# A fused convolution and two feed-forward layers: the first tile's tap sums move from VectorE to TensorE

## The chip, the cores and the metric

The kernel runs on one core of one Trainium2 chip. The metric is the device time of one execution in microseconds (us), lower is better. A profiled execution also gives a span: the time from its first to its last instruction.

## What is computed

Two batches of 4096 rows with 192 channels go through a causal convolution whose seven weights are drawn for each row and each of eight heads (24 channels a head) and pass a softmax first. The result goes through two feed-forward layers of width 2048, the first with a squared ReLU, the second with `h * cos(h)`.

```python
w = exp(weight_gen - max(weight_gen, -1)); w = w / (sum(w, -1) + 1e-09)
out = np.einsum('bshk,bskhg->bshg', w, x_unf)   # x_unf: rows s-6 .. s of x, by head
x = out.reshape(8192, 192)
h = np.maximum(x @ w_in, 0.0);  x = h * h @ w_out      # first layer
h = x @ w_in2;  out = (h * np.cos(h)) @ w_out2          # second layer
```

## The kernel before

**Tiles and slots.** The 8192 tokens are worked off in 16 tiles of 512 (`TILES`, `TOK`). A tile has 16 slots (`SLOTS`), one for each 128 columns of the hidden width, so slot `n` runs from 0 to 255. The program is written out without loops on the chip: each engine has its own list of instructions, and semaphores order the engines among themselves. What stands in these lists, and where, is set by hand, by tables such as `CONV_SLOTS` and `HI_AT`.

**Precision.** Each matrix is held as a high part in float32r (TensorE's reduced float32) and a low part that is the difference. A product is then three float32r matmuls (high by high, low by high, high by low). ScalarE makes the high parts, VectorE or GpSimd the low ones. The 192 channels are split into 128 (part 0, names with `a`) and 64 (part 1, names with `d`). Most matmuls are issued as two halves, for the upper and the lower 64 rows of the array (`TOP`, `BOTTOM`, `tile 64*128` in the profile).

**The first tile's convolution** is the place of the change. On VectorE, `convolve_first` multiplies seven shifted windows of `xc` (4 rows by 192 channels = 768 elements a partition) by the weights in `gen` and adds the products up in `x1`. The seven products go by turns into four buffers: the two halves of `tap`, `relu` and `wave` (its tile is shown as `turns`). The last tap is split by channels so that part 0 is done first. TensorE has nothing to compute in this time: it runs transpositions of the identity, `keep_busy` (L621), in counts that follow VectorE's steps, then turns the finished sum with `turn_x1` (L702: 8 transpositions of 64 rows for each part) into two PSUM tiles, part 0 into `y1` and part 1 into `y2`. The semaphore `x1_turned` tells ScalarE, which makes `xa_hi` and `xd_hi` (L1245); VectorE makes `xa_lo` and `xd_lo` (L1531).

**Around it.** In the head ScalarE makes the high parts of the first four weight pieces (`piece_his`, L1100) ahead of `xa_hi`; the other twelve follow at the end of slots given by `HI_AT`. VectorE makes the low parts of piece 0 (L1523, L1527) after `convolve_first`; when both are there (`piece_ready[0]`, 2), GpSimd starts on the low parts of all other pieces (L554 to L560). SyncE loads the pieces into a ring of four stage buffers, and the rows of the second tile (`load_rows(1)`, L450) once `first_product` says that the last product has been made.

**The slots of the head.** Slots 0 to 2 are one block each (`up_alone`, six matmuls); slots 3 to 17 (`head_slot`) interleave the product into the hidden layer with the product out of it for the slot three before, for which they wait for `g1_ready`: VectorE's low part `g_lo` (L1486). In `ACT_SQUARES` ScalarE does the squaring, in the other slots VectorE. VectorE also computes the second tile's convolution (`convolve_second`, L1360 and L1369: 7 products and 6 sums) behind the work of the slots in `CONV_SLOTS`, and softmax steps behind the slots in `SOFTMAX_AFTER`. After slot 13 TensorE turns the second tile. From slot 19 on both layers run together.

Of the kernel before, what the change touches and what calls it, by code (L numbers as in the profile page):

```python
# [7 lines left out]
def conv_ffn_ffn_kernel(nc, x_d, gen_d, w_in1_d, w_out1_d, w_in2_d, w_out2_d, out_dram):  # L8
# [103 lines left out]
    with ctx:  # L112
# [82 lines left out]
        first_sum = sem("first_sum")  # L195
# [52 lines left out]
        LATE = 4  # L248

        ACT_SQUARES = (2, 3, 4, 5, 6, 7, 8)  # L250
        CONV_SLOTS = (1, 1, 2, 2, 3, 4, 5, 6, 7, 8, 9, 10, 11)
# [3 lines left out]
        HI_AT = {4: 2, 5: 4, 6: 5, 7: 6, 8: 8, 9: 9, 10: 11, 11: 13, 12: 15, 13: 18, 14: 20, 15: 22}  # L255
# [94 lines left out]
        def turn_banks(t, part):  # L350

            return y2 if (t, part) == (0, 1) else y1

# [242 lines left out]
        def _(pe):  # L596
# [91 lines left out]
            def down_d(down, side, k, start=False, stop=False):  # L688

                y, l, f, hi, lo = down  # L690
                return half(y[:, 1, :], wo[l][:, f, DA:2 * P], lo if k == 1 else hi, side, start=start and f == 0,
                            stop=stop and f == SLOTS - 1)

# [335 lines left out]
            def head_slot(t, i, par, o, down):  # L1029
# [31 lines left out]
                if (t, i) == (0, turn_at(0)):  # L1061
                    pe.wait_ge(x1_ready, 1)
# [18 lines left out]
            turn_x1(0, 1)  # L1081
# [8 lines left out]
        def _(act):  # L1090
# [180 lines left out]
        def _(dve):  # L1271
# [100 lines left out]
            def convolve_first():  # L1372

                weights = gen[:, 0:JJ * GEN].rearrange("p (r k) -> p r k", k=TAPS)
                flat = [tap[:, 0, :], tap[:, 1, :],
                        relu[:, :, :].rearrange("p b n -> p (b n)")[:, 0:JJ * DM],
                        wave.rearrange("p b n -> p (b n)")[:, 0:JJ * DM]]
                total = x1[:, 0:JJ * DM]
# [4 lines left out]

                def product(k):
                    if k >= 4:
                        dve.wait_ge(first_sum, k - 4 + (k == 4))
                    tap_k = last - k
                    dve.tensor_tensor(flat[k % 4].rearrange("p (r g) -> p r g", g=GROUP),
                                      xc[:, tap_k * DM:(tap_k + JJ) * DM].rearrange("p (r g) -> p r g", g=GROUP),
                                      weights[:, :, tap_k:tap_k + 1].to_broadcast([P, JJ * HEADS, GROUP]),  # L1390
                                      ALU.mult).then_inc(first_product, 1)

                def last_product(a, b):
                    by_head = [v.rearrange("p (j h g) -> p j h g", j=JJ, g=GROUP)[:, :, a:b, :]
                               for v in (flat[last % 4], xc[:, 0:JJ * DM])]
                    of_heads = gen[:, 0:JJ * GEN].rearrange("p (j h k) -> p j h k", j=JJ, k=TAPS)[:, :, a:b, 0:1]
                    dve.wait_ge(first_sum, last - 4)
                    dve.tensor_tensor(by_head[0], by_head[1], of_heads.to_broadcast([P, JJ, b - a, GROUP]),
                                      ALU.mult).then_inc(first_product, 1)

                def channel_sum(k, a, b):
# [171 lines left out]
```

## Time and profile before

| | |
|---|---|
| median of 3 runs | 1182.05 us (1182.01 to 1182.32) |
| the profiled execution | 1182.28 us |
| its span | 1180.5 us |
| TensorE busy, share of the span | 1163.7 us, 99% |
| VectorE | 965.2 us, 82% |
| ScalarE | 807.2 us, 68% |
| GpSimd | 366.9 us, 31% |

The profiled execution took 1.8 us more than its span, which lie before its first and behind its last instruction. It stands 0.23 us above the median of the runs. Engines are named PE (TensorE's matmuls), PEld (its weight loads, which overlap them), DVE (VectorE), ACT (ScalarE), POOL (GpSimd) and SP (SyncE); L1388 is line 1388 of the kernel. The end of a matmul is modelled, so that TensorE counts as busy in short waits too; the starts of its instructions say more than its busy time.

### The profile page before, as it was taken

How to read it: one execution, taken by the hardware profiler on the slowest of the kernel's cores; microseconds unless marked ns; L12 is line 12 of the kernel's file. 1: busy time of each engine (PE TensorE's matmuls, PEld its weight loads, DVE VectorE, ACT ScalarE, POOL GpSimd, SP SyncE). 2: the span in 40 equal slices, each digit the busy share in tenths (PEclk: the TensorE clock that was granted, in tenths of full speed). 3: DMA queues.
4: the chain of work that ended last, by engine and by line, in shares of the span. 5: the costliest groups of instructions: out<-in, count | busy, mean ns of one | idle time of the engine just before them, and what ended most of it. 6: DMA issues, size and time to landing. Idle time of an engine off the chain costs nothing.

```text
span 1180.5 us, 25485 instructions
## 1 busy us (share of the span) xinstructions
PE 1163.7 (99%) x9800; PEld 1120.5 (95%) x9800; DVE 965.2 (82%) x1506; ACT 807.2 (68%) x1467; POOL 366.9 (31%) x265
## 2 busy tenths in 40 slices
PE   6999999999999999999999999999999999999998
PEld 5889999999999999999999999999999999999976
DVE  7978899978878787787878878787787878878787
ACT  4887666767666676676766666676676667666675
POOL 3995524070430706125070430705115070000000
PEclk9999999999999999999999999999999999999999
DMA  7512111011111101111011111101111000100000
GB/s 188 140 50 48 35 28 35 15 27 27 24 35 28 35 9 20 34 28 34 15 19 34 24 35 28 35 9 21 34 28 34 14 16 4 25 2 14 1 15 15
DMA packets 113173, 37.32 MB, mean 32 GB/s; under 512 B 101662, under 2 KB 110878, under 8 KB 113052
## 3 DMA queue, kind: packets, MB, share of 16 engines
q1 hardware_dynamic: 111100, 34.87, 14.1%
q8 instruction: 79, 1.29, 0.5%
q10 hardware_dynamic: 1952, 0.80, 0.3%
q14 instruction: 42, 0.34, 0.1%
HBM read 23.84 MB, written 6.29 MB: 26 GB/s over the span
## 4 chain that ended last, share of the span: by engine, by line
PE 92%; POOL 3%; DVE 2%; ACT 1%; issue 1%; SPq 0%; DMA 0%; POOLq 0%; ACTq 0%; DVEq 0%
PE y L600 48%; PE h L600 43%; POOL wd_lo L556 1%; POOL wa_lo L554 1%; POOL wo L560 1%; POOL wo L558 0%; DVE x L1414 0%; DMA xc<-in_x_dram 0%; POOL gen L540 0%; DVE turns L1323 0%; ACT relu L1116 0%; DVE x L1403 0%; DVE xd_lo L1510 0%; DVE g_lo L1328 0%; DVE h L1335 0%
## 5 line engine op out<-in xcount | busy, mean ns | idle before, releaser
L600 PE MATMUL y<-g_hi,wo 64*128 64x512 f32 x3048 | 693.0, 393 | 0.2
L600 PE MATMUL y<-g_lo,wo 64*128 64x512 f32 x2032 | 514.3, 392 | 0.0
L600 PEld LDWEIGHTS y<-g_hi,wo 64*128 64x128 f32 x3048 | 412.5, 184 | 16.3 <-PE y L600 4.9
L521 POOL TENSOR_TENSOR tap<-xc,gen 128x768 f32<-128x768 f32 x98 | 151.0, 1547 | 575.1 <-DVE xd_lo L1492 559.3
L600 PEld LDWEIGHTS y<-g_lo,wo 64*128 64x128 f32 x2032 | 295.6, 184 | 1.9
L1141 ACT ACTIVATE turns<-turns 128x512 f32<-128x512 f32 x238 | 150.5, 633 | 182.6 <-DVE turns L1443 182.6
L600 PE MATMUL h<-xa_hi,wa_hi 64*128 64x512 f32 x1018 | 264.7, 395 | 0.6 <-DVE g_lo L1486 0.4
L600 PE MATMUL h<-xa_lo,wa_hi 64*128 64x512 f32 x1018 | 262.8, 393 | 0.4 <-DVE g_lo L1328 0.3
L600 PE MATMUL h<-xa_hi,wa_lo 64*128 64x512 f32 x1018 | 261.5, 391 | 0.0
L1463 DVE TENSOR_TENSOR h<-h,turns 128x512 f32<-128x512 f32 x238 | 165.7, 696 | 114.9 <-ACT turns L1141 114.5
L1437 DVE SCALAR_TENSOR_TENSOR h<-h,relu 128x512 f32<-128x512 f32 x249 | 173.4, 696 | 56.6 <-ACT relu L1116 54.2
L1154 ACT ACTIVATE g_hi<-h 128x512 fp32r<-128x512 f32 x238 | 142.9, 600 | 86.8 <-DVE h L1463 86.8
L1116 ACT ACTIVATE relu<-h 128x512 f32<-128x512 f32 x256 | 152.8, 597 | 65.6 <-PE h L600 65.0
L1473 DVE SCALAR_TENSOR_TENSOR g_lo<-h,g_hi 128x512 fp32r<-128x512 f32 x238 | 164.7, 692 | 19.1 <-ACT g_hi L1154 0.9
L1486 DVE TENSOR_TENSOR g_lo<-h,g_hi 128x512 fp32r<-128x512 f32 x256 | 174.4, 681 | 1.6 <-issue 0.7
L1443 DVE SCALAR_TENSOR_TENSOR turns<-h,turns 128x512 f32<-128x512 f32 x238 | 162.3, 682 | 0.9 <-ACT turns L1126 0.5
L1166 ACT ACTIVATE g_hi<-relu 128x512 fp32r<-128x512 f32 x256 | 158.3, 618 | 0.4
L600 PEld LDWEIGHTS h<-xa_lo,wa_hi 64*128 64x128 f32 x1018 | 147.9, 184 | 3.7 <-DVE g_lo L1328 1.6
L600 PEld LDWEIGHTS h<-xa_hi,wa_lo 64*128 64x128 f32 x1018 | 148.1, 184 | 0.7
L1126 ACT ACTIVATE turns<-h 128x512 int32<-128x512 f32 x238 | 141.8, 596 | 1.4 <-PE h L600 1.4
L600 PEld LDWEIGHTS h<-xa_hi,wa_hi 64*128 64x128 f32 x1018 | 128.6, 184 | 12.5 <-issue 2.2
L600 PE MATMUL h<-xd_hi,wd_hi 64*128 64x512 f32 x513 | 132.6, 392 | 0.0
(122 smaller groups left out, 1067.1 us busy)
## 6 DMA issues: line engine op xcount, KB each, us to landing
xc<-in_x_dram SPq DMA_DIRECT2D x60, 240.0 KB
out_dram<-arena SPq DMA_DIRECT2D x62, 64.0 KB, 1.9
xt_a<-x_blocks SPq DMA_DIRECT2D x224, 16.0 KB, 1.8
arena<-in_moe_w_out_dram SPq DMA_DIRECT2D x16, 192.0 KB, 3.3
arena<-in_moe_w_in_dram SPq DMA_DIRECT2D x16, 128.0 KB, 2.6
out_dram<-arena SPq DMA_DIRECT2D x62, 32.0 KB, 1.7
xt_d<-x_blocks SPq DMA_DIRECT2D x112, 16.0 KB, 1.8
arena<-in_moe_w_in_dram SPq DMA_DIRECT2D x16, 64.0 KB, 2.9
```

The source lines that it names most:

```text
L521: pool.tensor_tensor(tap[:, k % 2, :].rearrange("p (r g) -> p r g", g=GROUP), rows[k], wk, ALU.mult).then_inc(pool_step, 1)
L600: return pe.matmul(o, w[rows, :], x[rows, :], start=start, stop=stop)
L1116: act.activation(relu[:, b, :], h1_bank(n), ACT.Relu).then_inc(relu_done, 1)
L1126: act.activation(turns[:, c, :], h2[c], ACT.Copy, bias=0.25).then_inc(turns_ready, 1)
L1141: act.activation(wave[:, c, :], wave[:, c, :], ACT.Sin, scale=2.0 * math.pi).then_inc(cos_ready, 1)
L1154: act.activation(g2_hi[:, c, :], h2[c], ACT.Copy, scale=2.0 * math.pi).then_inc(g2_hi_ready, 1)
L1166: act.activation(g1_buffers(n)[0], relu[:, n % 2, :], ACT.Square).then_inc(g1_hi_ready, 1)
L1437: dve.scalar_tensor_tensor(h1_bank(n), h1_bank(n), 0.0, relu[:, b, :], ALU.max, ALU.mult).then_inc(square_ready, 1)
L1443: dve.scalar_tensor_tensor(wave[:, c, :], h2[c], 0.25, turns[:, c, :], ALU.add, ALU.subtract).then_inc(fraction_ready, 1)
L1463: dve.tensor_tensor(h2[c], h2[c], wave[:, c, :], ALU.mult).then_inc(g2_made, 1)
L1473: dve.scalar_tensor_tensor(g2_lo[:, c, :], h2[c], 2.0 * math.pi, g2_hi[:, c, :], ALU.mult, ALU.subtract).then_inc(g2_ready, 1)
L1486: dve.tensor_tensor(lo, h1_bank(n), hi, ALU.subtract).then_inc(g1_ready, 1)
```

## The change

1. VectorE no longer adds in the first tile: `convolve_first` makes only the products (eight instructions in place of fifteen; the last tap is still split into the first 144 and the last 48 channels). It waits for `first_taken`, which TensorE raises when a tap's buffer has been read.
2. TensorE sums: `sum_x1` multiplies each product block by the identity with true float32 operands and accumulates the seven taps in PSUM, 16 matmuls for a tap, in place of `turn_x1` for this tile and of 55 of the `keep_busy` transpositions. 18 `keep_busy` transpositions are issued as soon as the first softmax maximum is there.
3. ScalarE makes the last of piece 2's and all of piece 3's high parts behind `xa_hi` and `xd_hi`.
4. `CONV_SLOTS` starts the second tile's convolution in slot 3 in place of slot 1 and ends it in slot 10 in place of 11, with two steps a slot up to slot 7. `HI_AT` moves pieces 4 to 7 from slots 2, 4, 5, 6 to slots 4, 5, 6, 7.

```diff
-        CONV_SLOTS = (1, 1, 2, 2, 3, 4, 5, 6, 7, 8, 9, 10, 11)
-        HI_AT = {4: 2, 5: 4, 6: 5, 7: 6, 8: 8, 9: 9, 10: 11, 11: 13, 12: 15, 13: 18, 14: 20, 15: 22}
+        WARM_UP = 18
+        CONV_SLOTS = (3, 3, 4, 4, 5, 5, 6, 6, 7, 7, 8, 9, 10)
+        HI_AT = {4: 4, 5: 5, 6: 6, 7: 7, 8: 8, 9: 9, 10: 11, 11: 13, 12: 15, 13: 18, 14: 20, 15: 22}
...
+            def sum_x1(k, part):
+
+                for jj in range(JJ):
+                    at = jj * DM + part * DA
+                    for side in range(2):
+                        rows = slice(side * DD, (side + 1) * DD)
+                        o = turn_banks(0, part)[0:DD if part else P, side, part * TOK // 2:(part + 1) * TOK // 2].rearrange(
+                            "p (q j n) -> p j q n", j=JJ, n=BLOCK)
+                        x = first_buffer(k)[rows, at:at + (DD if part else DA)]
+                        last = pe.matmul(o[:, jj], x, ident[rows, rows], start=k == 0 and jj == 0,
+                                         stop=k == TAPS - 1 and jj == JJ - 1)
+                return last
...
-            for k in range(2):
+            pe.wait_ge(gen_max[0], 1)
+            keep_busy(WARM_UP)
+            for k in range(TAPS):
                 pe.wait_ge(first_product, k + 1)
-                keep_busy(8 - k)
-            for k in range(1, TAPS - 2):
-                pe.wait_ge(first_sum, k)
-                keep_busy(8)
-            keep_busy(6)
-            pe.wait_ge(first_sum, TAPS - 1)
-            turn_x1(0, 0)
-            keep_busy(2)
-            pe.wait_ge(first_sum, TAPS + 1)
-            pe.wait_ge(pad_zeroed, 1)
-            turn_x1(0, 1)
+                last = sum_x1(k, 0)
+                if k == TAPS - 1:
+                    last.then_inc(x1_turned, 1)
+                    pe.wait_ge(first_product, k + 2)
+                last = sum_x1(k, 1)
+                last.then_inc(x1_turned if k == TAPS - 1 else first_taken, 1)
...
-            for pc in range(RING):
+            for pc in range(2):
                 for op in range(3):
                     piece_his(pc, op)
+            for op in range(2):
+                piece_his(2, op)
             for part in range(2):
                 act.wait_ge(x1_turned, part + 1)
                 act.activation(by_half(x1_high(0, part)), x1_source(0, part), ACT.Copy).then_inc(x1_hi_ready, 1)
+            piece_his(2, 2)
+            for op in range(3):
+                piece_his(3, op)
...
+                dve.wait_ge(x_own, FIRST_OWN)
+                product(0, 0, HEADS)
+                dve.wait_ge(x_loaded, FIRST_X)
+                for k in range(1, last):
                     if k >= 4:
+                        dve.wait_ge(first_taken, k - 3)
+                    product(k, 0, HEADS)
+
+                dve.wait_ge(first_taken, last - 3)
+                product(last, 0, wide)
+                product(last, wide, HEADS)
```

The order of the instructions shows it at three places. On VectorE, the first tile's convolution, before (`tap`, `relu` and `turns` are the product buffers, `x` is the sum `x1`):

```order
L1388 TENSOR_TENSOR relu<-xc,gen 128x768
L1414 TENSOR_TENSOR x<-tap 128x768
L1388 TENSOR_TENSOR turns<-xc,gen 128x768
L1414 TENSOR_TENSOR x<-x,relu 128x768
L1388 TENSOR_TENSOR tap<-xc,gen 128x768
L1414 TENSOR_TENSOR x<-x,turns 128x768
L1388 TENSOR_TENSOR tap<-xc,gen 128x768
L1414 TENSOR_TENSOR x<-x,tap 128x768
L1398 TENSOR_TENSOR relu<-xc,gen 128x4x144
L1403 TENSOR_TENSOR x<-x,tap 128x4x128
L1398 TENSOR_TENSOR relu<-xc,gen 128x4x48
L1403 TENSOR_TENSOR x<-x,relu 128x4x128
```

And in the changed kernel, the whole of it with the four instructions behind it:

```order
L1408 TENSOR_TENSOR tap<-xc,gen 128x768 x2
L1408 TENSOR_TENSOR relu<-xc,gen 128x768
L1408 TENSOR_TENSOR turns<-xc,gen 128x768
L1408 TENSOR_TENSOR tap<-xc,gen 128x768 x2
L1408 TENSOR_TENSOR relu<-xc,gen 128x4x144
L1408 TENSOR_TENSOR relu<-xc,gen 128x4x48
L1516 TENSOR_TENSOR wa_lo<-arena,wa_hi 128x256
L1520 TENSOR_TENSOR wd_lo<-arena,wd_hi 64x256
L1524 TENSOR_TENSOR xa_lo<-y,xa_hi 128x512
L1524 TENSOR_TENSOR xd_lo<-y,xd_hi 64x512
```

All sums are gone, and the low parts of weight piece 0 follow the last product at once. On TensorE, from the program's start to the first matmul of slot 0, before:

```order
L621 MATMUL h<-ident 128x128 x53
L702 MATMUL y<-ident,x 128x2x32 x8
L621 MATMUL h<-ident 128x128 x2
L702 MATMUL y<-ident,x 128x2x32 x8
L628 MATMUL h<-xa_hi,wa_hi 128x512
```

and in the changed kernel:

```order
L628 MATMUL h<-ident 128x128 x18
L711 MATMUL y<-ident,tap 128x2x32 x8
L711 MATMUL y<-ident,tap 64x2x32 x8
L711 MATMUL y<-ident,tap 128x2x32 x8
L711 MATMUL y<-ident,tap 64x2x32 x8
L711 MATMUL y<-ident,relu 128x2x32 x8
L711 MATMUL y<-ident,relu 64x2x32 x8
L711 MATMUL y<-ident,turns 128x2x32 x8
L711 MATMUL y<-ident,turns 64x2x32 x8
L711 MATMUL y<-ident,tap 128x2x32 x8
L711 MATMUL y<-ident,tap 64x2x32 x8
```

(two more taps of 16 matmuls follow before slot 0). The last place is VectorE in slots 3 to 5 of the changed kernel, where `tap` and `y` belong to the second tile's convolution, `stat` to the softmax and `g_lo` is what TensorE waits for:

```order
L1384 TENSOR_TENSOR tap<-xc,gen 128x768 x2
L1300 TENSOR_REDUCE stat<-gen 128x64
L1479 TENSOR_TENSOR g_lo<-h,g_hi 128x512
L1393 TENSOR_TENSOR y<-tap 128x768
L1384 TENSOR_TENSOR tap<-xc,gen 128x768
L1300 TENSOR_REDUCE stat<-gen 128x64
L1479 TENSOR_TENSOR g_lo<-h,g_hi 128x512
L1393 TENSOR_TENSOR y<-y,tap 128x768
L1384 TENSOR_TENSOR tap<-xc,gen 128x768
L1300 TENSOR_REDUCE stat<-gen 128x64
```

Before, the first four of the convolution's steps stood behind slots 1 and 2, and from slot 3 on each slot had one. The lists of GpSimd and SyncE are the same in both kernels.

## Rows read from the trace of the kernel before

**Rows 1.** The page: busy time of two engines, and the chain that ended last.

```profile
PE 1163.7 (99%) x9800; PEld 1120.5 (95%) x9800; DVE 965.2 (82%) x1506; ACT 807.2 (68%) x1467; POOL 366.9 (31%) x265
PE 92%; POOL 3%; DVE 2%; ACT 1%; issue 1%; SPq 0%; DMA 0%; POOLq 0%; ACTq 0%; DVEq 0%
```

**Rows 2.** Timeline of VectorE, 0 to 24 us: start, time, instruction, idle before.

```profile
6.73 0.96 DVE L1388 TENSOR_TENSOR tap<-xc,gen 128x768 f32<-128x768 f32 x1
8.25 0.96 DVE L1388 TENSOR_TENSOR tap<-xc,gen 128x768 f32<-128x768 f32 x1 [0.57 <-DMA xc<-in_x_dram]
9.13 0.95 DVE L1388 TENSOR_TENSOR relu<-xc,gen 128x768 f32<-128x768 f32 x1
10.00 0.95 DVE L1414 TENSOR_TENSOR x<-tap 128x768 f32<-128x768 f32 x1
...
16.08 0.75 DVE L1398 TENSOR_TENSOR relu<-xc,gen 128x576 f32<-128x576 f32 x1
16.75 0.69 DVE L1403 TENSOR_TENSOR x<-x,tap 128x512 f32<-128x512 f32 x1
17.35 0.35 DVE L1398 TENSOR_TENSOR relu<-xc,gen 128x192 f32<-128x192 f32 x1
...
19.61 0.42 DVE L1527 TENSOR_TENSOR wd_lo<-arena,wd_hi 64x256 fp32r<-64x256 f32 x1
20.06 0.69 DVE L1531 TENSOR_TENSOR xa_lo<-y,xa_hi 128x512 fp32r<-128x512 f32 x1
```

**Rows 3.** Timeline of TensorE's matmuls, 7 to 24 us.

```profile
18.36 0.46 PE L702 MATMUL y<-ident,x 64*128 64x64 f32 x8 [0.40 <-DVE x L1403]
...
19.61 0.50 PE L628 MATMUL h<-xa_hi,wa_hi 128*128 128x512 f32 x1
...
20.80 0.50 PE L635 MATMUL h<-xa_lo,wa_hi 128*128 128x512 f32 x1
...
21.81 0.39 PE L600 MATMUL h<-xd_lo,wd_hi 64*128 64x512 f32 x1
```

**Rows 4.** Timeline of TensorE's weight loads, 7 to 14 us: the idle-time transpositions.

```profile
7.80 3.00 PEld L621 LDWEIGHTS h<-ident 128*128 128x128 f32 x15 [7.80 <-issue]
11.00 0.86 PEld L621 LDWEIGHTS h<-ident 128*128 128x128 f32 x8 [0.21 <-DVE x L1414]
```

**Rows 5.** Timeline of ScalarE, 0 to 24 us.

```profile
17.08 0.51 ACT L1100 ACTIVATE wo<-arena 128x384 fp32r<-128x384 f32 x1
18.87 0.60 ACT L1245 ACTIVATE xa_hi<-y 128x512 fp32r<-128x512 f32 x1 [1.27 <-PE y L702]
19.73 0.59 ACT L1245 ACTIVATE xd_hi<-y 64x512 fp32r<-64x512 f32 x1 [0.26 <-PE y L702]
22.24 0.60 ACT L1116 ACTIVATE relu<-h 128x512 f32<-128x512 f32 x1 [1.92 <-PE h L600]
```

**Rows 6.** Windows: us, busy and count of PE, PEld, DVE, ACT, POOL, clock, DMA.

```profile
44.00:48.00 4.00, 4.00 (x33) 3.67 (x30) 3.96 (x6) 3.33 (x7) 3.73 (x4) 1.00 0.56 164
```

**Rows 7.** Timeline of weight loads, 24 to 84 us: the same load in slots 9 and 10; the stall.

```profile
33.82 0.18 PEld L600 LDWEIGHTS h<-xa_hi,wa_hi 64*128 64x128 f32 x1 [0.78 <-DVE g_lo L1486]
...
41.39 0.18 PEld L600 LDWEIGHTS h<-xa_hi,wa_hi 64*128 64x128 f32 x1
...
43.96 0.18 PEld L600 LDWEIGHTS h<-xa_hi,wa_hi 64*128 64x128 f32 x1
```

**Rows 8.** Timeline of VectorE, 20 to 84 us: convolution, softmax and low part in the head.

```profile
31.62 1.37 DVE L1360 TENSOR_TENSOR tap<-xc,gen 128x768 f32<-128x768 f32 x1
...
35.51 0.94 DVE L1360 TENSOR_TENSOR tap<-xc,gen 128x768 f32<-128x768 f32 x1
36.37 0.61 DVE L1276 TENSOR_REDUCE stat<-gen 128x64 f32<-128x448 f32 x1
36.90 0.68 DVE L1486 TENSOR_TENSOR g_lo<-h,g_hi 128x512 fp32r<-128x512 f32 x1
```

**Rows 9.** Timeline of GpSimd, 20 to 84 us.

```profile
20.11 0.73 POOL L554 TENSOR_TENSOR wa_lo<-arena,wa_hi 128x256 fp32r<-128x256 f32 x1 [17.53 <-DVE wd_lo L1527]
...
27.66 1.27 POOL L556 TENSOR_TENSOR wd_lo<-arena,wd_hi 64x256 fp32r<-64x256 f32 x1
...
30.73 1.45 POOL L554 TENSOR_TENSOR wa_lo<-arena,wa_hi 128x256 fp32r<-128x256 f32 x1
```

More of the change, by code:

```diff
@@ L194, in conv_ffn_ffn_kernel @@
         first_product = sem("first_product")
-        first_sum = sem("first_sum")
+        first_taken = sem("first_taken")
         pool_step = sem("pool_step")
@@ L352, in turn_banks, with first_buffer @@
             return y2 if (t, part) == (0, 1) else y1
+        def first_buffer(k):
+            return [tap[:, 0, :], tap[:, 1, :], relu[:, :, :].rearrange("p b n -> p (b n)")[:, 0:JJ * DM],
+                    wave.rearrange("p b n -> p (b n)")[:, 0:JJ * DM]][k % 4]
         def x1_source(t, part):
@@ L1061, in head_slot @@
                 if (t, i) == (0, turn_at(0)):
+                    pe.wait_ge(pad_zeroed, 1)
                     pe.wait_ge(x1_ready, 1)
@@ L1372, in convolve_first @@
             def convolve_first():
[L1374 to L1378, printed above, removed]
                 last = TAPS - 1
                 wide = -(-DA // GROUP)
-                def product(k):
-                    if k >= 4:
[L1386 to L1399, printed above, removed]
@@ L1401, in channel_sum @@
-                def channel_sum(k, a, b):
-                    sums, more = [v.rearrange("p (j d) -> p j d", j=JJ)[:, :, a:b] for v in (total, flat[k % 4])]
-                    dve.tensor_tensor(sums, sums, more, ALU.add).then_inc(first_sum, 1)
-                dve.wait_ge(x_own, FIRST_OWN)
-                product(0)
-                dve.wait_ge(x_loaded, FIRST_X)
-                product(1)
-                for k in range(1, last - 1):
-                    product(k + 1)
-                    dve.wait_ge(first_product, k + 1)
-                    if k >= 2:
-                        dve.wait_ge(first_sum, k - 1)
-                    dve.tensor_tensor(total, flat[0] if k == 1 else total, flat[k % 4],
-                                      ALU.add).then_inc(first_sum, 1)
@@ L1417, in convolve_first @@
-                last_product(0, wide)
-                dve.wait_ge(first_product, last)
-                dve.wait_ge(first_sum, last - 2)
-                channel_sum(last - 1, 0, DA)
-                last_product(wide, HEADS)
-                dve.wait_ge(first_product, last + 1)
-                dve.wait_ge(first_sum, last - 1)
-                channel_sum(last, 0, DA)
-                channel_sum(last - 1, DA, DM)
-                dve.wait_ge(first_product, last + 2)
-                dve.wait_ge(first_sum, last + 1)
@@ L1428, in convolve_first, with product @@
-                channel_sum(last, DA, DM)
+                def product(k, a, b):
+                    tap_k = last - k
+                    to, rows = [v.rearrange("p (j h g) -> p j h g", j=JJ, g=GROUP)[:, :, a:b, :]
+                                for v in (first_buffer(k), xc[:, tap_k * DM:(tap_k + JJ) * DM])]
+                    weights = gen[:, 0:JJ * GEN].rearrange("p (j h k) -> p j h k", j=JJ, k=TAPS)
+                    dve.tensor_tensor(to, rows, weights[:, :, a:b, tap_k:tap_k + 1].to_broadcast([P, JJ, b - a, GROUP]),
+                                      ALU.mult).then_inc(first_product, 1)
```

## The prediction

> **What bounds the kernel now.** I read the page first: TensorE is busy for 99% of the span and carries 92% of the chain that ended last [rows 1]. So in the steady part only matmuls count, and this change removes none there. What it can move is the time at which that part begins. The timelines of the first 24 us show this stretch: VectorE runs without a gap from 8.25 us to beyond 19 us, seven products and their sums of 0.87 us each by their starts [rows 2], and the first matmul of slot 0 stands at 19.61 [rows 3]. From slot 3 on the same weight load comes every 2.57 us (41.39 and 43.96), with one stall of 0.78 us at 33.8, put down to `g_lo` of VectorE [rows 7]. In this stretch TensorE issues 33 half matmuls in 4.00 us, one each 0.121 us, and VectorE is busy for 3.96 of the 4 [rows 6]. So an earlier slot 0 is worth its full amount at the end, less what VectorE then fails to follow. A measurement of this kernel can tell about 0.2% (2.4 us) from no change.
>
> **The products, without the sums.** VectorE's first product ends at 7.69 (6.73 + 0.96); the second has to wait for rows of `x` and starts at 8.25 [rows 2]. The others follow at 0.87 us, which is the distance of the starts 9.13 and 10.00. With only products left, products 2 to 6 end at 9.21, 10.08, 10.95, 11.82 and 12.69, the first part of the last (0.75 us) at about 13.35, its second part at 13.65. TensorE's wait is then on these.
>
> **The sums on TensorE.** A tap is 16 float32 matmuls of 64 columns. The trace has no float32 product; it has its neighbour, the transposition of the same block by the same identity: 8 in 0.46 us with the last one's end of 0.22 us in it [rows 3], thus one each 31 to 34 ns, upper and lower half side by side. That is the bound from below. Bound from above: nothing side by side, each product as dear as two 128-wide transpositions at 0.86 / 8 = 0.107 us [rows 4], 214 ns. I take 61 ns, twice the neighbour. The product has the neighbour's operands, halves and output; what it adds is the multiplication of full float32 values, which I price as the neighbour once again, since it is nearer to that row than to one which uses all 128 rows of the array. 61 ns is also what 256 columns of a half matmul cost in the head (0.121 us for 512 [rows 6]).
>
> The Trainium skill says in "FP8 and Floating Point Precision", section "TensorE Precision Notes", that true float32 takes four passes through the array. As an estimate from it: four passes of 64 columns are 256 columns, 61 ns at the head's rate; if each pass costs a whole transposition's 31 ns, 124 ns, and the sum below would be +2.2 us in place of -3.8. No run shown here has such a product.
>
> At 61 ns a tap takes 0.98 us, a little more than VectorE's 0.87. Tap 0 runs from 7.75 to 8.73; tap 1 waits for its product and runs from 9.27; then they stand back to back: tap 5 ends at 14.17, part 0 of tap 6 at 14.66, part 1 at 15.15. With 0.2 us for the last matmul's end, `xa_hi` starts on ScalarE at 14.9 instead of 18.87 [rows 5]: **4.0 us earlier**. VectorE's waits for `first_taken` come to nothing: product 4 needs tap 0's buffer (8.9), it would start at 10.87 anyway; products 5 and 6 need 10.4 and 11.4, for starts at 11.73 and 12.60.
>
> **Slot 0.** Before, `xa_lo` started only at 20.06, behind `wd_lo` (19.61) [rows 2], though `xa_hi` had ended at 19.47. Now both low parts of piece 0 are made from 13.65 to 14.6, ahead of it, so `xa_lo` starts at 15.55 and the third matmul at about 16.3 instead of 20.80 [rows 3]. `xd_hi` follows at 15.45 to 16.05, `xd_lo` ends at 16.85, and the last matmul of the slot starts at about 17.1 instead of 21.81: another 0.7 us. The first `relu` of 22.24 [rows 5] comes at 17.5: **4.7 us earlier**. ScalarE's four moved copies (0.31 to 0.41 us by their starts, about 1.45 us) fit between 16.05 and 17.5, and the last of them used to end at 17.59 [rows 5], so their data is there.
>
> **The clock.** The first 15 transpositions took 3.00 us, 200 ns each; the next 8 took 0.86 us, 107 ns each [rows 4]. The first were at TensorE's lower level of 1.2 GHz, the next at 2.4 GHz, though nothing but transpositions had run since 7.80; the clock column of the windows prints 1.00 everywhere and does not show it. Now 18 of them start at 3.8, when the first maximum is ready, and end at 3.8 + 18 x 0.21 = 7.6, just before tap 0. The rise came by 3.2 us after the first; here that is by 7.0. I cost the clock at nothing; the cover is these 3.8 us.
>
> **SyncE and GpSimd.** The second tile's rows were issued at the end of the last product (17.70); they now stand behind the second softmax load, from about 14.3 on, and are needed only in slot 3, at about 26. GpSimd's list starts after `wd_lo`: at 14.6 instead of 20.11 [rows 9]. Both are worth nothing: none of TensorE's waits of the head was put down to GpSimd. Piece 4's high part moves from slot 2 to slot 4, so GpSimd can start on it at about 29 and has it by 32.5; TensorE wants it in slot 8, at 34. The cover is 1.5 us.
>
> **VectorE in slots 3 to 10.** Here something is paid back. The second tile's convolution now begins two slots later and ends one earlier. In slots 3 to 7 VectorE has in each slot `g_lo` (0.60 by starts), two steps of the convolution (2 x 0.87) and one maximum (0.53), 2.87 us against TensorE's 2.57. That is 1.5 us of lag after five slots. A product can also be stretched while GpSimd runs: one took 1.37 us and a like one 0.94, and GpSimd's `wd_lo` and `wa_lo` took 1.27 and 1.45 us beside 0.73 [rows 8, 9]. With 0.4 us more on three to five products the lag is 2.7 to 3.6 us. TensorE bears 2.6 us of it: a slot's `g_lo` is made 2.5 us after the slot (relu, square, low part), and wanted two slots, 5.14 us, after it. So stalls of 0 to 2.1 us come in slots 9 to 13 (the upper end has all seven products stretched and ScalarE's copies in five slots running late). Against it stands the stall of 0.78 us at 33.8, which goes, since the `g_lo` of slot 3 no longer waits behind the convolution. I take a net loss of 0.9 us; the bounds are a gain of 0.8 and a loss of 2.1.
>
> The Trainium skill, "SBUF — State Buffer", section "Who interferes with whom", has the rule that a VectorE tensor_tensor with two SBUF inputs and a GpSimd read shut each other out, the later one waiting for the whole of the first. The rows 1.37 against 0.94 agree that there is a price but show only half a product of it, so the sum keeps 0.4 us; by the rule it would be up to 0.95 for each, and the loss would pass 2.1 us.
>
> **The sum**: 4.7 - 0.9 = 3.8 us less. The profiled execution of 1182.28 us stands 0.23 us over the median of 1182.05, so I forecast 1182.05 - 3.8 = **1178.3 us**. A product's price moves this by 0.088 us a ns (taps 1 to 5 and half of tap 6, 88 matmuls behind 9.27), from 95 ns on by 0.104 (tap 0 then outlasts 9.27, and 104 matmuls stand behind 7.75): the gain falls under 0.2% at 77 ns, is gone at 103 ns, and turns to a loss over 0.2% at 126 ns.
>
> **Rivals.**
> - *TensorE becomes the bound of the sum.* The passes of a product, or its two halves, do not run side by side: 124 ns (four times the transposition's spacing) gives part 0 done at 7.75 + 104 x 0.124 = 20.6 instead of 14.6: -3.8 + 6.0 = +2.2, 1184.2 us. For it: if a product is several passes, they all go to one half before the other half's follow, where the transpositions alternate. Against it: with 512 columns the halves do overlap all through the head [rows 6]. Prices from 77 to 126 ns, chance 0.25, all within 0.2%.
> - *Slower.* The same place, the price at its upper bound: 214 ns, 3.4 us a tap, part 0 done at 7.75 + 104 x 0.214 = 30.0, 15.4 us after my 14.6: -3.8 + 15.4 = +11.6, 1193.6 us. It decides against the change from 126 ns on. Against it: halves would have to lose all overlap, which no row shows. Chance 0.14, and 0.02 for a new wait behind the moved steps.
> - *VectorE's lag eats the gain.* Stretched products in all slots: 2.1 us or more lost, 1179.5 to 1180.5 us. Chance 0.07, within 0.2%.
> - *The low clock stays during the first taps.* If the transpositions did not count, tap 0 and most of tap 1 would run at 1.2 GHz, at double price, until about 3 us after 7.75: tap 1 ends at 11.1 in place of 10.25, 0.9 us lost, 1179.2 us, still faster. Chance 0.06. The Trainium skill, "TensorE: Matmul & The Clock Gate", Part 4, says that transpose mode does not count as busy for the clock; the halved times of rows 4 speak against it.
>
> **How the numbers follow.** My forecast has 0.46. Faster: 0.46 + 0.06 = 0.52. Within 0.2%: 0.25 + 0.07 = 0.32. Slower: 0.16. The range starts at 1176.8: VectorE is the bound at its 0.87 us (a price of 54 ns or less), 5.5 us won at the first `relu`, 0.3 lost. It ends at 1184.3, which takes in the first rival at 124 ns and leaves out the slower case.
>
> **What would show it.** Right: taps of about 1 us on TensorE from 7.75 on, `xa_hi` near 14.9, the first `relu` near 17.5, then slots of 2.57 us with at most a microsecond of waits for `g_lo` around slots 9 to 13. Wrong: VectorE waiting for TensorE between products, groups of 8 sums that take 0.8 us or more, transpositions still at 200 ns when tap 0 begins, or waits of TensorE for GpSimd's low parts in slot 8.

## The result, and the profile after

| | before | changed |
|---|---|---|
| median, us | 1182.25 (7 runs, 1181.89 to 1182.39) | 1193.15 (7 runs) |
| its runs, us | one group | 1183.70, 1183.91; 1193.02, 1193.15, 1193.49, 1193.68, 1193.91 |
| ratio | | 1.0071, interval 1.0048 to 1.0094 |
| profiled execution, us (span) | 1182.28 (1180.5) | 1183.70 (1181.9) |

The forecast was 1178.3, range 1176.8 to 1184.3: the median lies outside, on the side of the slower rival. (The ratio goes by all runs of both kernels; that of the two medians is 1.0092.) The runs of the changed kernel fall into two groups 9.7 us apart, which are followed one by one below: the lower (1183.8, +1.6 us) is the one that was profiled, the upper (1193.5, +11.2 us) has no trace of its own.

The page's busy times, and its chain by engine:

```profile
PE 1170.1 (99%) x9971; PEld 1124.2 (95%) x9971; DVE 959.8 (81%) x1498; ACT 805.5 (68%) x1467; POOL 364.9 (31%) x265
PE 94%; POOL 2%; ACT 2%; DVE 1%; issue 1%; DMA 0%; ACTq 0%; POOLq 0%
```

Against [rows 1] TensorE has 6.4 us more of work and VectorE 5.4 us less. The timeline of TensorE's matmuls, 3 to 24 us (columns as in [rows 3]):

```profile
3.88 3.83 PE L628 MATMUL h<-ident 128*128 128x128 f32 x18 [3.88 <-DVE stat L1300]
7.74 3.37 PE L711 MATMUL y<-ident,tap 64*128 64x64 f32 x64
11.04 1.72 PE L711 MATMUL y<-ident,relu 64*128 64x64 f32 x32
12.69 1.72 PE L711 MATMUL y<-ident,turns 64*128 64x64 f32 x32
14.34 3.37 PE L711 MATMUL y<-ident,tap 64*128 64x64 f32 x64
17.64 1.72 PE L711 MATMUL y<-ident,relu 64*128 64x64 f32 x32
19.54 0.47 PE L635 MATMUL h<-xa_hi,wa_hi 128*128 128x512 f32 x1 [0.18 <-ACT xa_hi L1266]
...
20.32 0.48 PE L642 MATMUL h<-xa_lo,wa_hi 128*128 128x512 f32 x1
...
21.31 0.39 PE L607 MATMUL h<-xd_lo,wd_hi 64*128 64x512 f32 x1
```

The seven taps stand back to back, 1.65 us from one start to the next (11.04, 12.69, 14.34). Each shows 32 matmuls, not 16: a float32 product is recorded as two loads and two matmuls. So a product costs 1.65 / 16 = 0.103 us. By form, the groups of weight loads in 7 to 20 us (busy us, mean ns of one):

```profile
L711 PEld LDWEIGHTS y<-ident,tap 64*128 64x128 f32 x64 | 3.9, 187 | 0.5 <-DVE tap L1408 0.3
L711 PEld LDWEIGHTS y<-ident,tap 64*64 64x64 f32 x64 | 2.2, 134 | 0.3
```

The loads of part 0 (128 columns as weights) take 187 ns, those of part 1 (64) 134 ns. VectorE, 6 to 21 us:

```profile
6.73 0.96 DVE L1408 TENSOR_TENSOR tap<-xc,gen 128x768 f32<-128x768 f32 x1
7.95 0.96 DVE L1408 TENSOR_TENSOR tap<-xc,gen 128x768 f32<-128x768 f32 x1 [0.26 <-DMA xc<-in_x_dram]
...
12.81 1.03 DVE L1408 TENSOR_TENSOR relu<-xc,gen 128x576 f32<-128x576 f32 x2 [0.43 <-PE y L711]
...
14.28 0.42 DVE L1520 TENSOR_TENSOR wd_lo<-arena,wd_hi 64x256 fp32r<-64x256 f32 x1
19.43 0.69 DVE L1524 TENSOR_TENSOR xa_lo<-y,xa_hi 128x512 fp32r<-128x512 f32 x1 [4.73 <-ACT xa_hi L1266]
```

VectorE is through at 13.8 and with the low parts at 14.7, as foreseen, and then stands for 4.73 us: TensorE has become the bound of the sum. ScalarE's `xa_hi` starts at 18.80 (18.87 before, [rows 5]), the third matmul at 20.32 (20.80), the first `relu` at 21.74 (22.24). The start is won by 0.5 us, not 4.7. Two of the forecast's signs of being wrong are here: part 0's group of 8 sums takes 0.89 us, and VectorE waits for TensorE between products (0.43 us at 12.81).

Then it is paid back. TensorE's weight loads, 24 to 100 us, that waited for another engine's data in the second tile's slots:

```profile
43.80 0.18 PEld L607 LDWEIGHTS h<-xa_hi,wa_hi 64*128 64x128 f32 x1 [1.00 <-DVE g_lo L1479]
47.04 0.18 PEld L607 LDWEIGHTS h<-xa_hi,wa_hi 64*128 64x128 f32 x1 [0.85 <-DVE g_lo L1479]
49.92 0.18 PEld L607 LDWEIGHTS h<-xa_hi,wa_hi 64*128 64x128 f32 x1 [0.49 <-DVE g_lo L1479]
52.71 0.18 PEld L607 LDWEIGHTS h<-xa_hi,wa_hi 64*128 64x128 f32 x1 [0.40 <-DVE g_lo L1479]
```

Together 2.7 us, at slots 9 to 12; the stall of 0.78 us at 33.8 [rows 7] is gone. VectorE is behind since the second tile's convolution; two of its rounds:

```profile
37.54 1.49 DVE L1384 TENSOR_TENSOR tap<-xc,gen 128x768 f32<-128x768 f32 x1
38.96 0.61 DVE L1300 TENSOR_REDUCE stat<-gen 128x64 f32<-128x448 f32 x1
39.49 0.67 DVE L1479 TENSOR_TENSOR g_lo<-h,g_hi 128x512 fp32r<-128x512 f32 x1
40.09 0.95 DVE L1393 TENSOR_TENSOR y<-y,tap 128x768 f32<-128x768 f32 x1
40.95 1.50 DVE L1384 TENSOR_TENSOR tap<-xc,gen 128x768 f32<-128x768 f32 x1
```

One such slot takes 40.95 - 37.54 = 3.41 us against TensorE's 2.57, with the product stretched from 0.94 [rows 8] to 1.49. Of the seven products, four took 1.37 to 1.50 us (34.26 to 44.36) and one 1.17. The `relu` starts give the account against before, us: slot 0 -0.50, slot 6 (35.89 against 36.72) -0.83, slot 10 (46.70, 46.99) -0.29, slot 11 +0.39, slot 13 (56.64, 55.15) +1.49, last slot +1.45. The two profiled executions differ by 1.42.

So three questions are left: whether the price of the products is the whole reason for the start, whether the lag comes from the slot tables alone, and what the upper group is.

### The profile page after: what moved, and what is told of

It is laid out like the page before. It is cut to its first block, busy times and chain, and to the rows that moved or that the text cites. A ratio compares the mean times of both kernels' runs of the same rounds, so it can differ in the third digit from the quotient of the medians.

```text
span 1181.9 us, 25812 instructions
## 1 busy us (share of the span) xinstructions
PE 1170.1 (99%) x9971; PEld 1124.2 (95%) x9971; DVE 959.8 (81%) x1498; ACT 805.5 (68%) x1467; POOL 364.9 (31%) x265
## 4 chain that ended last, share of the span: by engine, by line
PE 94%; POOL 2%; ACT 2%; DVE 1%; issue 1%; DMA 0%; ACTq 0%; POOLq 0%
PE y L607 49%; PE h L607 44%; PE y L711 1%; POOL wd_lo L563 0%; POOL wo L565 0%; POOL wo L567 0%; POOL wa_lo L561 0%; PE h L628 0%; ACT relu L1135 0%; POOL gen L547 0%; DVE turns L1347 0%; DMA gen<-in_weight_gen_dram 0%; DVE xd_lo L1503 0%; DVE g_lo L1352 0%; ACT gen L1124 0%
## 5 line engine op out<-in xcount | busy, mean ns | idle before, releaser
L607 PE MATMUL y<-g_lo,wo 64*128 64x512 f32 x2032 | 507.6, 392 | 0.0
L607 PEld LDWEIGHTS y<-g_hi,wo 64*128 64x128 f32 x3048 | 404.6, 184 | 17.0 <-PE y L607 4.9
L607 PEld LDWEIGHTS y<-g_lo,wo 64*128 64x128 f32 x2032 | 287.3, 184 | 2.5
L607 PE MATMUL h<-xa_hi,wa_hi 64*128 64x512 f32 x1018 | 260.9, 395 | 1.3 <-DVE g_lo L1479 1.0
L607 PE MATMUL h<-xa_lo,wa_hi 64*128 64x512 f32 x1018 | 258.8, 393 | 0.3 <-DVE g_lo L1352 0.3
L607 PE MATMUL h<-xa_hi,wa_lo 64*128 64x512 f32 x1018 | 257.3, 391 | 0.0
L607 PEld LDWEIGHTS h<-xa_lo,wa_hi 64*128 64x128 f32 x1018 | 144.0, 184 | 3.9 <-DVE g_lo L1352 1.7
L607 PEld LDWEIGHTS h<-xa_hi,wa_lo 64*128 64x128 f32 x1018 | 144.2, 184 | 0.9
```

The costliest lines, as they stand in the source:

```text
L607: return pe.matmul(o, w[rows, :], x[rows, :], start=start, stop=stop)
```

## The experiments

Where a kernel has two groups, lower is compared with lower, by their medians. On the chips of the experiments the kernel before had medians of 1181.85 to 1182.12.

### The change unaltered, with more runs

> The changed kernel once more, unaltered. Its runs fall in two groups, near 1183.8 and near 1193.4 us, 9.6 us apart. Theory C (clock): in the upper group TensorE's clock has not risen when the sums begin at 7.7 us, so that a tap takes 3.3 us in place of 1.65 and the seven taps end near 29 in place of 19.4. Rival S (elsewhere): the 9.6 us lie behind the head, in a late landing or a wait. C expects about 7 runs in 10 near 1193.4 and, if the profiled one is of that group, taps of 3.3 us and everything behind them shifted by one amount; S expects taps of 1.65 us in every profile.

Measured: eight runs of 1183.10 to 1183.93, two of 1193.45 and 1193.98; ratio 1.0031, interval 1.0008 to 1.0054. The two groups are there on another chip, in other shares (2 of 10 in the upper one, 5 of 7 in the result), and the median depends on the shares. The lower group's median is 1183.5 here.

The profiled run is of the lower group again, so it cannot decide between the two explanations of the upper one. But its first taps differ from those above:

```profile
3.91 4.07 PE L628 MATMUL h<-ident 128*128 128x128 f32 x18 [3.91 <-DVE stat L1300]
7.92 3.67 PE L711 MATMUL y<-ident,tap 64*128 64x64 f32 x64
```

The transpositions stand 0.213 us apart to the last one here, the pace of 1.2 GHz, and the first two taps last 3.67 us in place of 3.37: the products reach their faster pace only at about 8.6 us, inside the first tap. So the forecast's sign "transpositions still at 200 ns when tap 0 begins" is met in a run of the lower group. The first `relu` comes at 22.21: of the 0.5 us won at the start 0.03 is left. The time is the same all the same (1183.66 against 1183.70): the four waits for `g_lo` are as long as above, and the 0.5 us is made up where the third tile begins. There the change's profiled run waits 1.02 us for VectorE, and this one does not:

```profile
73.80 0.19 PEld L635 LDWEIGHTS h<-xa_hi,wa_hi 128*128 128x128 f32 x1 [1.02 <-DVE xd_lo L1503]
```

### Twice the idle transpositions

```diff
-        WARM_UP = 18
+        WARM_UP = 36
```

> 36 idle transpositions ahead of the sums in place of 18: they last from 3.9 to about 10 or 11 us, and the first sum begins there instead of at 7.7. C, if only the length of the stretch ahead matters: the clock is up before the first tap in every run, all runs in one group, the sums end 2.5 to 3.5 us later than in the profiled run of the change, 1186 to 1187.5 us. C with the addition that sums do not raise the clock and transpositions do only by chance: still two groups. S: two groups 9.6 us apart at the same share as before, both 3 us higher.

Measured: 1185.89 to 1186.84, one group. The taps run from 10.95 to 22.57 and the first `relu` comes at 24.94, 3.2 us later than in the change, and the time is 3.1 us more (1186.6 against 1183.5). None of the four runs lies near 1193, and what the start loses is lost at the end.

### The slot tables of before

```diff
-        CONV_SLOTS = (3, 3, 4, 4, 5, 5, 6, 6, 7, 7, 8, 9, 10)
+        CONV_SLOTS = (1, 1, 2, 2, 3, 4, 5, 6, 7, 8, 9, 10, 11)
-        HI_AT = {4: 4, 5: 5, 6: 6, 7: 7, 8: 8,
+        HI_AT = {4: 2, 5: 4, 6: 5, 7: 6, 8: 8,
```

> The change with the slot tables of before (CONV_SLOTS from slot 1, HI_AT with pieces 4 to 7 at slots 2, 4, 5, 6). Theory V (VectorE's lag): the three waits for g_lo near 43.8, 47.0 and 49.9 (2.3 us together) go, one of about 0.8 us may come back near slot 6, and the lower group falls from 1183.7 to 1181.8 to 1182.3. Rival L: the waits come from the whole of VectorE's work in the head and stay in another place; the lower group stays within 0.5 us of 1183.7.

Measured: nine runs of 1180.73 to 1181.69, one of 1191.06. Lower group 1181.3 against 1183.5: the tables cost 2.2 us. The three largest waits of TensorE's loads, 19 to 100 us, of this kernel (in total, times, longest):

```profile
PEld h L607 <- issue: 3.1, 10, 0.5
PEld h L635 <- issue: 1.4, 4, 0.4
PEld y L657 <- DVE g_lo L1479: 0.5, 1, 0.5
```

### The slot tables of the change, alone in the kernel before

The same two lines the other way round, in the kernel before.

> The kernel before with the change's two slot tables alone; its convolution as before, first relu unchanged near 22.2. Theory (VectorE's lag in slots 9 to 13 is from the tables, 2.0 to 2.3 us, and a start 0.5 us earlier hides none of it): 1183.8 to 1184.5, with PEld waits for g_lo of the second tile in slots 9 to 12. Rival (the tables pay where the head starts later and only the sums' new load on GpSimd and ScalarE makes the lag): 1181.6 to 1182.3, no such waits.

Measured: 1183.46 to 1184.37, median 1183.79 against 1182.12; ratio 1.0016, interval 1.0007 to 1.0025. Its largest wait in the same stretch:

```profile
PEld h L600 <- DVE g_lo L1486: 2.8, 4, 1.0
```

The same four waits, without a product on TensorE. The lag is the tables' alone, 1.7 us here and 2.2 us in the change; it is no price of an earlier start. Which of the two tables makes it was not tried.

### The products as transpositions

```diff
-                        last = pe.matmul(o[:, jj], x, ident[rows, rows], start=k == 0 and jj == 0,
-                                         stop=k == TAPS - 1 and jj == JJ - 1)
+                        last = pe.transpose(o[:, jj], x, ident[rows, rows])
```

This leaves the summing out: the first tile's `x1` is then its last tap alone.

> Each float32 product of the sums is issued as a transposition of the same block (nothing is accumulated: the result of the first tile is the last tap alone). Theory P (price): 16 of them take 0.5 to 0.6 us in place of 1.65, TensorE waits for VectorE, the first half of x is ready near 13.9 and xa_hi starts near 14.2 instead of 18.8; slot 0 ends 4.5 us or more earlier, and the time falls to about 1179 to 1180 us if the waits in slots 9 to 12 stay, with one group, since at a low clock the transpositions cost only 1 us a tap. Rival: the sums are held by something else than the price of a product (semaphore, PSUM bank); then a tap stays near 1.6 us.

Measured: 1178.15 to 1179.81, median 1178.47; ratio 0.9972, interval 0.9961 to 0.9983. TensorE's matmuls:

```profile
9.75 0.68 PE L711 MATMUL y<-ident,relu 64*128 64x64 f32 x16 [0.18 <-DVE relu L1407]
...
12.36 0.69 PE L711 MATMUL y<-ident,tap 64*128 64x64 f32 x16 [0.19 <-DVE tap L1407]
13.02 0.69 PE L711 MATMUL y<-ident,relu 64*128 64x64 f32 x16
14.60 0.47 PE L635 MATMUL h<-xa_hi,wa_hi 128*128 128x512 f32 x1 [0.89 <-ACT xa_hi L1265]
```

A tap of 16 transpositions takes 0.66 us (12.36 to 13.02), recorded as 16 matmuls, not 32, and TensorE waits for VectorE at nearly every tap; the first `relu` comes at 16.87, 4.87 us before the change's, and the time is 5.0 us less (1178.5 against 1183.5). With all else of the change in place, the price of the product is what kept the start from coming early. It also gives the row that the trace of before lacked: 0.66 / 16 = 41 ns a transposition in whole taps, where I had 31 to 34.

### No idle transpositions

```diff
-        WARM_UP = 18
+        WARM_UP = 0
```

> The change without any idle transposition ahead of the sums. Theory C (clock): sums of this kind do not raise TensorE's clock in the time they take, only what stood ahead of them did. Then every run has taps of 3.3 us, xa_hi starts near 30 and the time is 1193 to 1195 us in one group, which is the change's upper group made on purpose. Rival R: sums raise the clock like any work; then the first two taps are slow, the others 1.65 us, and the time is 1185.5 to 1187 us.

Measured: 1193.24, 1197.07, 1197.28, 1197.35. The profiled run is the one of 1193.24, at the level of the upper group:

```profile
7.83 5.96 PE L711 MATMUL y<-ident,tap 64*128 64x64 f32 x64 [7.83 <-DVE tap L1408]
13.73 3.02 PE L711 MATMUL y<-ident,relu 64*128 64x64 f32 x32
...
25.52 3.02 PE L711 MATMUL y<-ident,relu 64*128 64x64 f32 x32
28.46 0.79 PE L635 MATMUL h<-xa_hi,wa_hi 128*128 128x512 f32 x1
29.05 0.63 PE L638 MATMUL h<-xa_hi,wa_lo 128*128 128x512 f32 x1
...
31.22 0.39 PE L607 MATMUL h<-xd_hi,wd_lo 64*128 64x512 f32 x1
```

A tap takes 2.95 us, start to start, at the level of 1.2 GHz; the 512-column matmul that follows takes 0.63 us, and 0.39 from 31.22 on, which is 2.4 GHz. The sums ran without a gap from 7.83 to 28.5 and the level did not rise; it rose between 30.68 and 31.22, while the fourth matmul of 512 columns ran, behind the first three and three transpositions. (The clock column of the windows prints 1.00 all through this stretch; the change of pace shows the level.) So in this trace the sums do not bring the level, and in the change only the 18 transpositions ahead of them can; that every tap of the upper group then takes 2.95 us is inferred. Here the first `relu` comes at 31.88, 10.1 us after the change's, and the time is 9.7 us more than 1183.5: the distance of the groups. One group at 1193 to 1195 was expected; the three runs near 1197 have no trace, and what cost them 4 us more is open.

### 24 transpositions, from the start of TensorE's work

```diff
-            pe.wait_ge(gen_max[0], 1)
             keep_busy(WARM_UP)
```

with `WARM_UP = 24`.

> The change with 24 idle transpositions that start as soon as the identity is there (2.6 us) in place of 18 from 3.9 us; they end at the same time, 7.7 us, so no sum is later. C: a stretch 1.2 us longer catches the rise in more runs: at most 1 in 10 in the upper group near 1193.5, the others at 1183 to 1183.8. If the share of the upper group stays as it was (8 of 17), the length of the stretch is not what decides.

Measured: all 11 runs in 1182.98 to 1184.08; ratio 1.0012, interval 1.0004 to 1.0021. The transpositions run from 2.63 to 8.01, and the first tap starts 0.2 us later than in the change. The upper group is gone, at no cost. The upper group had 7 of the 17 runs so far (the expectation says 8). Over all kernels whose products have 128 and 64 weight columns by turns: with 18 transpositions (the change twice, with the old tables, and with five blocks, below) 11 of 39 runs lie 9 us or more above their lower group, with 24 or 36 of them none of 34. That is what a missed rise would do. The margin is small even so: read from the pace of the instructions, the rise came about 3 to 6 us after the first transposition in the 13 profiles that have them, and in this run about when the first product began. In the lower group of the change nothing was to be won by this, and nothing was.

### 64 columns by 64 throughout

Part 0's product of 128 columns is split in two; slot tables of before.

```diff
-                        x = first_buffer(k)[rows, at:at + (DD if part else DA)]
-                        last = pe.matmul(o[:, jj], x, ident[rows, rows], start=k == 0 and jj == 0,
-                                         stop=k == TAPS - 1 and jj == JJ - 1)
+                        for c in range(1 if part else 2):
+                            x = first_buffer(k)[rows, at + c * DD:at + (c + 1) * DD]
+                            oc = o[c * DD:(c + 1) * DD]
+                            last = pe.matmul(oc[:, jj], x, ident[rows, rows], start=k == 0 and jj == 0,
+                                             stop=k == TAPS - 1 and jj == JJ - 1)
```

> The change with the slot tables of before, and the 128 channels of part 0 summed as two products of 64 columns in place of one of 128: 24 products a tap in place of 16. In the changed kernel's trace a product with 128 weight columns takes 0.111 us, one with 64 takes 0.058, and 0.35 us a tap pass between the groups of 128 and of 64. Theory W (weight load in series with the pass for 128 columns, and a gap where the width changes): 24 x 0.058 = 1.4 us a tap and no gap, 0.25 us a tap less, 1179.3 to 1179.9 us in the lower group against 1181.2 of the run with the old tables. If column halves also run beside each other, 0.7 to 0.9 us a tap, VectorE is the bound and the time is 1176 to 1177.5 us. Rival: a product costs 0.1 us whatever its width, 2.5 us a tap, 1187 us or more.

Measured: seven runs of 1178.55 to 1179.76, five of 1183.77 to 1187.56. TensorE's rows where one tap gives way to the next:

```profile
11.47 0.27 PE L713 MATMUL y<-ident,turns 64*64 64x64 f32 x1
...
12.40 0.27 PE L713 MATMUL y<-ident,tap 64*64 64x64 f32 x1
```

By all runs the ratio is 0.9997: no gain. A tap is now 24 products in 0.93 us (11.47 to 12.40), 39 ns each, near to VectorE's 0.87. The 1176 to 1177.5 us that were expected for such taps did not come even in the lower group. So what was dear was not a float32 product as such, but the one with weights of 128 columns, and the change of width twice a tap. The profiled run is one of 1185.35; its windows from 16 us on (columns as in [rows 6]):

```profile
16.00:20.00 4.00, 2.72 (x30) 1.84 (x24) 1.38 (x2) 2.49 (x6) 3.86 (x7) 0.97 1.06 255
20.00:24.00 4.00, 4.00 (x9) 2.11 (x8) 2.73 (x6) 1.72 (x4) 3.57 (x7) 0.50 1.03 222
24.00:28.00 4.00, 4.00 (x15) 2.66 (x15) 3.14 (x5) 2.04 (x5) 0.61 (x1) 0.50 1.13 226
28.00:32.00 4.00, 4.00 (x17) 3.33 (x17) 3.19 (x3) 2.08 (x6) 2.74 (x3) 0.50 1.10 226
```

The level, up since the first products (8.0 us), falls between 19.6 and 19.9 us, and the first slots run at 0.50. Here it was lost, not missed (of the other four runs of the upper group there is no trace). And the sums have two holes without a visible releaser, one of 0.84 us at 13.74 and one in the last tap:

```profile
17.75 0.33 PE L713 MATMUL y<-ident,relu 64*64 64x64 f32 x3 [1.28 <-issue]
```

### VectorE adds two pairs of taps, TensorE sums five blocks

Slot tables of before.

```diff
+                def add(to, more, a, b):
+                    sums, others = [first_buffer(k).rearrange("p (j d) -> p j d", j=JJ)[:, :, a:b] for k in (to, more)]
+                    dve.tensor_tensor(sums, sums, others, ALU.add).then_inc(first_product, 1)
...
+                add(3, 4, 0, DM)
...
+                add(1, 2, 0, DA)
+                add(1, 2, DA, DM)
...
-            for k in range(TAPS):
-                pe.wait_ge(first_product, k + 1)
+            BLOCKS = ((0, 1), (1, 2), (2, 3), (3, 6), (1, 9))
+            for k, (_, made) in enumerate(BLOCKS):
+                pe.wait_ge(first_product, made)
```

> The change with the slot tables of before, and two of the six additions given back to VectorE (taps 3 and 4, and 5 and 6), so that TensorE sums five blocks in place of seven. Theory B (TensorE is the bound of the sum at 1.65 us a block): its last block is fed at 14.8 and part 0 is there at 15.8 in place of 19, 3 us earlier; 1178.3 to 1179 us in the lower group; in the upper group five blocks at 3.3 us, 6.6 us more. Rival: VectorE's waits for the buffers eat it, 1180 us or more.

Measured: nine runs of 1178.52 to 1180.44, three of 1189.47 to 1190.18. The sums end at 16.89 instead of 19.36, and the first `relu` comes at 19.27, 2.5 us before the change's; the lower group's median is 1178.85. By all runs the ratio is 0.9999. The upper group does not come out of the pace of the sums: five blocks at 2.95 in place of 1.65 us are 6.5 us more, and it lies 11.1 us above the lower one. It has no trace; what the other 4.6 us are is open.

### The two better kernels with the level held

The last two kernels with 24 early transpositions, and more between the sums: one behind each tap of the first and six behind its last, two and six in the second.

> The sums with products of 64 columns by 64 throughout, the slot tables of before, 24 transpositions from the start of TensorE's work (as in early24), one more behind each tap and six behind the last. Theory (only transpositions and 512-column matmuls hold the clock, products do not): the 2.4 GHz level stays from before the first tap to the first 512-column matmul, a tap takes about 0.93 us, first relu near 18.5 to 19.5, time 1177.5 to 1179.2 in all runs, no run near 1184. Rival (the sums lose the clock whatever stands between them): two groups as in quad, 1178.5 to 1179.8 and 1183.8 to 1187.6, and a granted clock of 0.50 in some stretch between 16 and 32 us. Second rival (the transpositions stand in the sums' way): one group near 1180.5.

> hybrid (VectorE adds two pairs of taps, TensorE sums five blocks, slot tables of before) with 24 early transpositions, two more behind each block and six behind the last. Theory: one group at hybrid's lower level, 1178.5 to 1179.5, the 1190 runs gone, first relu near 19.3. Rival (the clock is lost during the sums whatever stands between them): some runs remain near 1190.

Measured: the first 1179.39 to 1180.90 and one run of 1183.09, median 1180.42, ratio 0.9987 (0.9978 to 0.9996); the second 1179.76 to 1180.36 in all 11 runs, median 1179.96, ratio 0.9983 (0.9974 to 0.9992). No run lies at 1184 or above, but both are slower than expected (1177.5 to 1179.2 and 1178.5 to 1179.5), since the transpositions lie on the path: in the second the first `relu` comes at 20.70, 1.43 us later than without them. In the first the hole is there again, on the path in the last tap:

```profile
18.04 0.68 PE L713 MATMUL y<-ident,relu 64*64 64x64 f32 x15 [1.28 <-issue]
```

### Early transpositions alone

The kernel of five blocks with the 24 early transpositions and none between.

> hybrid with the 24 early transpositions alone, none between the blocks and none behind the last. Theory (the level of 2.4 GHz is missed at the start or not at all; once it is there the sums of five blocks, 9 us long, do not lose it): one group at hybrid's lower level, 1178.3 to 1179.3, 1.0 to 1.5 us below hybrid_warm, whose 16 added transpositions lie on the path. Rival (in hybrid the level is lost during the sums, and the transpositions between the blocks were what held it): runs near 1184 to 1190 come back.

Measured: seven runs of 1178.47 to 1179.17 and one of 1184.52, median 1178.71; ratio 0.9971, interval 0.9960 to 0.9983: by its median the fastest kernel that does the whole sum, 3.4 us below before, with one run in eight above before. The one run of 1184.52 is the profiled one, and shows the level lost during the sums:

```profile
12.95 1.72 PE L711 MATMUL y<-ident,turns 64*128 64x64 f32 x32 [0.19 <-DVE turns L1413]
15.41 2.73 PE L711 MATMUL y<-ident,tap 64*128 64x64 f32 x32 [0.74 <-DVE tap L1413]
```

```profile
12.00:16.00 4.00, 3.07 (x60) 2.66 (x60) 3.97 (x6) 1.62 (x5) 0.00 (x0) 0.97 0.77 226
16.00:20.00 4.00, 4.00 (x34) 3.31 (x32) 1.82 (x4) 2.41 (x6) 3.23 (x6) 0.50 1.07 233
```

A block of the same size takes 1.72 us at the upper level and 2.73 us as the level falls. The theory's time was met in seven runs, the rival's in one.

## Why the prediction was wrong

- **The product's price** failed, and with it the forecast. "I take 61 ns, twice the neighbour": it measured 103 ns on average. In its lower group, which lies inside the range, the kernel is the first rival, TensorE as the bound of the sum, though not by halves that don't overlap: part 0's eight products stand at 111 ns each, part 1's eight at 58, and the rest of the 1.65 us (1.65 - 0.89 - 0.46 = 0.30) is at the two changes of width. My 61 was right for part 1; I took both parts as equal, though part 0's weights have 128 columns, and left out the switches. The four passes that the Trainium skill gives a true float32 product ("FP8 and Floating Point Precision", section "TensorE Precision Notes") made an estimate of 61 ns too, by their columns; part 1's 58 agrees with it, part 0's 111 does not come out of it.
- **The working from a price to the start** holds: at 103 ns it puts `xa_hi` at about 18.7, and it came at 18.80, 0.07 us earlier than before. The forecast called 103 ns neutral for the whole time, and that failed: at this price the lower group is 1.6 us slower, for the smaller win in slot 0 and the larger lag below.
- **Slot 0** was right in kind: the low parts made ahead win 0.43 us beyond `xa_hi` (0.50 - 0.07; 0.7 was said). So was the schedule of VectorE (13.8 against 13.65). The products as transpositions put the first `relu` at 16.87 where 17.5 was forecast.
- **VectorE's lag** was right in place and cause, and too small: net 1.95 us (from -0.50 to +1.45) against 0.9, within its bounds of -0.8 to 2.1. "0.4 us more on three to five products": it was 0.43 to 0.56 on four and 0.23 on a fifth, and 2.87 us a slot became 3.41. I argued the lag as the price of an earlier start; the tables alone in the kernel before cost 1.7 us.
- **The clock** was the second failure, and it sets the median. "I cost the clock at nothing; the cover is these 3.8 us": the 18 transpositions were a cover in 2 of 7 runs and in 8 of 10. The step that failed is "The rise came by 3.2 us after the first; here that is by 7.0": one trace's delay was taken as fixed, and over the profiles it was about 3 to 6 us; in the kernel with the old tables the level rose only at about 9.0 us, some 1.1 us after the first product had begun. The rival on this had the right place, a low level during the taps, but its reason (transpositions don't count) is refuted, and its price was wrong: "until about 3 us after 7.75", 0.9 us, assumed that the sums themselves would bring the rise. They did not in the one trace that shows it: without the transpositions it comes 23 us after 7.83. The whole sum runs at 2.95 us a tap, and 0.9 us became 9.7. The Trainium skill's rule in "TensorE: Matmul & The Clock Gate", Part 4, that transpose mode does not count, I had set against [rows 4]; here the trace does not agree with the rule: transpositions are what raises the level (24 of them ahead of the change's sums in all 11 runs), and plain float32 products did not.
- **The slower rival** gave 1193.6 us and the median is 1193.15. That is a coincidence: it had the products at 214 ns for a loss of overlap. In the upper group they would be 2.95 / 16 = 184 ns, for the clock. That the upper group of the change itself has this pace is inferred, from the kernel without transpositions that ran at 1193.24 and from the kernels with more of them that have no such group; no run of the change at 1193 was profiled.

**The account.** Lower group: start -0.50, lag +1.95, sum +1.45, measured +1.42 between the profiled executions. (In the second profile of the change it is start -0.03, lag +1.97, and -0.5 at the third tile, for the same sum.) Upper group: 9.7 more. **Left open:** what makes the level fall during the sums in some runs (two were seen, one of the kernel of 64 by 64 and one of the last kernel, both with gaps of 0.7 us and more between their taps, but the kernel of 64 by 64 with transpositions between kept it over a hole of 1.28 us) while the change's own back-to-back taps kept it in every profiled run; what the upper group of the kernel of five blocks has beyond its sums; and the holes of 0.84 and 1.28 us.

## What to carry to other kernels

An operation that no row shows deserves a probe before a schedule is built on it, priced in the shape it will have: here one product with 64 weight columns cost 58 ns and its twin with 128 cost 111, with 0.15 us for a switch between them. Work that is moved to an engine whose clock depends on its past needs that clock secured by something other than the work itself, and a kernel that gets it by a narrow margin shows it as two groups of runs, which a single profile does not tell. And schedule tables that are changed "to match" are a change of their own: tried alone, these were a loss of 1.7 us.

## What was not expected of the hardware

- TensorE's level of 2.4 GHz rose after idle transpositions of 128 columns alone, and in the one trace without them did not rise in 20.7 us of unbroken float32 products of 64 columns, but came once the 512-column matmuls had begun.
- The same 18 transpositions did not bring the rise at a fixed time: it came at about 7.4 us in the change, at about 8.6 us when it was run again and at about 9.0 us with the old tables, the last two with the products already running.
- A float32 product is recorded as two loads and two matmuls. At 2.4 GHz, upper and lower half in turn: 111 ns with 128 weight columns, 58 ns with 64, 39 ns where four quarters of the array take turns.
- TensorE stood for 1.28 us in the last tap with no releaser that the profile shows, in both kernels of 64 by 64 products.
